# Attention with V as the stationary operand and P divided on GpSimd; expert stage with projections, values and three pieces of wo @ w1 between its units

## The chip, the cores and the metric

The kernel runs on one core of one Trainium2 chip. The time is device microseconds of that core for one execution, from the launch of the program to its end. PE is the matrix engine (TensorE), PEld its weight loads, DVE the vector engine, ACT the scalar engine, POOL is GpSimd, SP the engine whose queue issues all the DMAs here. PSUM is the memory that PE writes, SBUF the other on-chip memory; GpSimd reads SBUF alone.

## The reference

Three layers follow one another: a sparse attention with 8 heads, a mixture of 4 experts (each one causal head of attention, two experts for each position), and a block that mixes positions at rank 32 and then runs a wide two-layer network.

```python
# B, H, S, D = 2, 8, 768, 64
scores = q @ k.T / sqrt(D) + bias            # keys kept: the first n_global = 8 and the last n_local = 96
a = softmax(scores); x = a @ v               # x: 2 x 768 x 512
# experts: E = 4, K = 2 kept, head of 64
logits = x @ w_gate; w = softmax over the two largest
for e in range(E):
    a = causal_softmax((x @ wq[e]) @ (x @ wk[e]).T / 8)
    out += w[e] * (a @ (x @ wv[e]) @ wo[e])
# last block
u = out + (U V along the positions)
result = u + relu(u @ w_ch1) @ w_ch2
```

## The kernel before, in words

All of it is written out by hand: each engine has one program, in the order in which it is written, and semaphores are the only links. An engine that waits holds everything behind it.

**First attention.** 8 pairs of heads (p) times 6 tiles of 128 queries (i) are 48 units u. Two units are a duo d, so 24 duos, three to a pair. A unit has two halves s (the two heads, `par`). A half takes 128 queries against at most 256 keys: the tile's own 128 and a block of 128 made of the first 32 keys and the last 96 of the tile before. The steps are: `scores` on PE (line 1002 for tiles 0 and 1, lines 1004 and 1005 for 32 and 224 keys of the others), `attend` on DVE (L655: adds the bias, scales, keeps the minimum, writes `prob`), the exponential on ACT (`exp_step`, L460), `inverse` on DVE (1 / sum), `transposes` of P on PE (L1019, into `ps_t`), `evac` of the transposed P on ACT (L469), `values` on PE (L1038: P stationary, 64 columns of V moving, into `ps_o`), `scale_out` on DVE (L679, times 1 / sum), `x_turn` on PE (L1046, transposes back), `x_out` on DVE (L690 and L692, x as a rounded part `xh` and a rest `xl`). The loops of the engines run over d and hold their lag in their indices:

```python
# PE                                   # DVE                        # ACT
scores(2d), scores(2d+1)               x_out(d-4)                   evac(2d-2), evac(2d-1)
transposes(2d-2), transposes(2d-1)     scale_out(d-3)               four exp of duo d
values(d-2)                            four attend of duo d
x_turn(d-3)                            inverse(d-1)
```

SP loads each pair's q and k (two buffers, so pair p waits until all the scores of pair p-2 are done) and its V. Behind pair 2 come the weights; `load_weights(2)` and `load_weights(3)` wait until GpSimd has made the low parts `wqk_l` of what lay in their buffer before (`wl_done`).

**Expert stage.** wo is transposed on PE (L1174). `project(pp)` makes k and q of one pair of experts for one batch (pp = 0 to 3) with matmuls of split operands (L985, three products each); `project_hi` on ACT and `project_lo` on DVE write k as `mkh` + `mkl` and q as `mqs`, and SP copies halves of them to the other partitions. `project_values` makes all 12 tiles of values before the first unit. 24 units v = 6 pp + i follow, unit i with i + 1 tiles of keys: `m_scores` (L1130), `m_attend` (DVE, L655), `m_exp` (ACT, L460), `m_normalise` (DVE, L700 to L711), `m_transposes` (PE, L1146), `mevac` (ACT, L517), `m_values` (PE, L1162). PE runs scores two units ahead. `project(1)` to `project(3)` come whole, after units 0, 6 and 12.

**Last block.** `natural` (L1210) turns the experts' output, `both_weights(j)` makes wo @ w1 in 8 pieces between the small steps of the mixing, and from 298 us on `hidden` and `second` run over 2 x 16 tiles of the wide network.

## Time and profile before

| | |
|---|---|
| three runs | 520.68, 529.01 and 536.24 us, median 529.01 |
| profiled execution | 521.91 us, of which the span of the trace is 520.1 |
| PE busy | 483.1 us (93%) |
| DVE, ACT, POOL busy | 228.5, 187.6, 80.2 us (44%, 36%, 15%) |
| granted TensorE clock | 0.98 of full speed |
| DMA | 34.54 MB, 66 GB/s |

The page gives for each engine the time in which at least one instruction ran. 1.8 us of the profiled time lie around the span. The stages of the span: first attention to 117 us, experts to 265 us, preparation of the last block to 298 us, the wide network to the end.

### The profile page before, as it was taken

How to read it: one execution, taken by the hardware profiler on the slowest of the kernel's cores; microseconds unless marked ns; L12 is line 12 of the kernel's file. 1: busy time of each engine (PE TensorE's matmuls, PEld its weight loads, DVE VectorE, ACT ScalarE, POOL GpSimd, SP SyncE). 2: the span in 40 equal slices, each digit the busy share in tenths (PEclk: the TensorE clock that was granted, in tenths of full speed). 3: DMA queues.
4: the chain of work that ended last, by engine and by line, in shares of the span. 5: the costliest groups of instructions: out<-in, count | busy, mean ns of one | idle time of the engine just before them, and what ended most of it. 6: DMA issues, size and time to landing. Idle time of an engine off the chain costs nothing.

```text
span 520.1 us, 8734 instructions
## 1 busy us (share of the span) xinstructions
PE 483.1 (93%) x3368; PEld 420.2 (81%) x3368; DVE 228.5 (44%) x710; ACT 187.6 (36%) x485; POOL 80.2 (15%) x57
## 2 busy tenths in 40 slices
PE   2999999989996888978799999999999999999997
PEld 1888888869984776857589988888888788888886
DVE  3477766643479658375815512222222212222212
ACT  1676777733044557456833311111111211111112
POOL 0023300000005200050025201111122101111110
PEclk9999999988998999979999999999999999999999
DMA  6946333002015020130021101111111113211103
GB/s 224 288 120 202 113 113 113 1 1 62 1 27 164 33 61 2 32 112 1 2 82 42 39 23 41 42 42 40 42 42 41 42 38 84 81 62 42 40 1 121
DMA packets 20842, 34.54 MB, mean 66 GB/s; under 512 B 5216, under 2 KB 8160, under 8 KB 20800
## 3 DMA queue, kind: packets, MB, share of 16 engines
q1 hardware_dynamic: 20800, 33.97, 21.9%
q8 instruction: 27, 0.44, 0.3%
q14 instruction: 15, 0.12, 0.1%
HBM read 27.67 MB, written 3.15 MB: 59 GB/s over the span
## 4 chain that ended last, share of the span: by engine, by line
PE 84%; DVE 8%; ACT 3%; issue 3%; DMA 1%; SPq 0%; DVEq 0%; ACTq 0%
PE ps_s L985 25%; PE ps_o L985 16%; PE ps_t L985 13%; PE ps_o L1038 7%; PE ps_t L1019 5%; PE ps_o L1162 3%; PE ps_s L1005 3%; PE ps_t L1146 3%; DVE prob L655 3%; PE ps_s L1130 2%; PE ps_s L1004 2%; ACT prob L460 1%; PE ps_s L1002 1%; PE ps_o L1046 1%; ACT probT L517 1%
## 5 line engine op out<-in xcount | busy, mean ns | idle before, releaser
L610 ACT ACTIVATE hidh<-ps_o 128x768 fp32r<-128x768 f32 x32 | 26.0, 812 | 181.4 <-PE ps_o L985 181.4
L460 ACT ACTIVATE prob<-prob,smin 128x256 f32<-128x256 f32 (+3 forms) x144 | 77.2, 543 | 28.0 <-DVE smin L655 28.0
L968 DVE SCALAR_TENSOR_TENSOR hidl<-ps_o,hidh 128x768 fp32r<-128x768 f32 x32 | 30.6, 958 | 95.0 <-ACT hidh L610 95.0
L419 POOL TENSOR_TENSOR fl<-fraw,fh 128x512 fp32r<-128x512 f32 x32 | 41.3, 1291 | 177.6 <-DVE fh L897 177.6
L985 PE MATMUL ps_s<-hidh,fl 128*128 128x512 f32 x128 | 50.5, 394 | 0.0
L985 PE MATMUL ps_s<-hidl,fh 128*128 128x512 f32 x128 | 50.2, 392 | 0.0
L985 PE MATMUL ps_s<-hidh,fh 128*128 128x512 f32 x128 | 50.1, 391 | 0.0
L897 DVE CAST fh<-fraw 128x512 fp32r<-128x512 f32 x32 | 13.6, 426 | 71.5 <-PE ps_t L985 71.5
L985 PE MATMUL ps_o<-xl,w01h 128*128 128x256 f32 (+1 forms) x128 | 43.3, 338 | 0.0
L985 PE MATMUL ps_o<-xh,w01h 128*128 128x256 f32 (+1 forms) x128 | 43.2, 338 | 0.0
L985 PE MATMUL ps_o<-xh,w01l 128*128 128x256 f32 (+1 forms) x128 | 43.1, 337 | 0.0
L1146 PE MATMUL ps_t<-ident,prob 128*128 128x128 f32 x168 | 26.6, 293 | 16.3 <-DVE prob L711 8.2
L1146 PEld LDWEIGHTS ps_t<-ident,prob 128*128 128x128 f32 x168 | 19.6, 149 | 21.6 <-DVE prob L711 10.0
L1038 PE MATMUL ps_o<-vN,probT 128*128 128x64 f32 x224 | 37.0, 276 | 0.0
L985 PE MATMUL ps_t<-hidh,fh 128*128 128x256 f32 x128 | 36.1, 282 | 0.0
L985 PE MATMUL ps_t<-hidl,fh 128*128 128x256 f32 x128 | 36.0, 281 | 0.0
L985 PE MATMUL ps_t<-hidh,fl 128*128 128x256 f32 x128 | 35.7, 279 | 0.0
L469 ACT ACTIVATE probT<-ps_t 128x512 f32<-128x512 f32 (+1 forms) x48 | 25.4, 560 | 27.3 <-PE ps_t L1019 26.9
L655 DVE CUSTOM_DVE_ANT_0 prob<-ps_s,bias 128x256 f32<-128x256 f32 (+1 forms) x96 | 32.9, 397 | 3.5 <-PE ps_s L1005 3.1
L517 ACT ACTIVATE probT<-ps_t 128x512 f32<-128x512 f32 (+3 forms) x64 | 25.6, 448 | 23.8 <-PE ps_t L1146 23.6
L655 DVE CUSTOM_DVE_ANT_0 prob<-ps_s,causal 128x128 f32<-128x128 f32 (+5 forms) x48 | 28.0, 620 | 9.3 <-PE ps_s L1130 9.1
L1038 PEld LDWEIGHTS ps_o<-vN,probT 128*128 128x128 f32 x224 | 31.4, 196 | 0.0
(175 smaller groups left out, 1096.1 us busy)
## 6 DMA issues: line engine op xcount, KB each, us to landing
fraw<-in_w SPq DMA_DIRECT2D x32, 256.0 KB, 2.6
wraw<-in_w SPq DMA_DIRECT2D x8, 512.0 KB, 3.7
qT<-in_q SPq DMA_DIRECT2D x8, 384.0 KB, 3.2
kT<-in_k SPq DMA_DIRECT2D x8, 384.0 KB, 3.8
vN<-in_v SPq DMA_DIRECT2D x8, 384.0 KB, 4.8
out<-prob SPq DMA_DIRECT2D x12, 256.0 KB, 2.6
vB<-in_v SPq DMA_DIRECT2D x8, 192.0 KB, 5.0
mkh<-mkh SPq DMA_DIRECT2D x8, 192.0 KB, 2.6
```

The lines of the kernel that those rows point to most:

```text
L419: return pool.tensor_tensor(lo, raw, hi.bitcast(F32), ALU.subtract)
L460: act.activation(prob_s, prob_s, ACT.Exp, bias=smin[:, col:col + 1], scale=-1.0, accum_out=ssum[:, col:col + 1]).then_inc(done, 1)
L469: act.activation(a_probT[u % 4][:, :, 0:w], ps_t[:, u % 2, 0:2 * w].rearrange("p (a n) -> p a n", a=2), ACT.Copy).then_inc(evac_done, 1)
L517: act.activation(probT[:, v % 2, par, j0 * P:j1 * P], ps_t[:, g % 2, 0:(j1 - j0) * P], ACT.Copy).then_inc(mevac_done, 1)
L610: act.activation(hidh[:, f % 2, :], ps_o[:, 0:S], ACT.Relu).then_inc(hidh_done, 1)
L655: dve.tensor_tensor_reduce(out=dst, in0=src, in1=mask, scale=-SCALE, scalar=3e38, op0=ALU.add, op1=ALU.min, accum_out=smin[:, col:col + 1] ...
L968: dve.scalar_tensor_tensor(hidl[:, f % 2, :], ps_o[:, 0:S], 0.0, hidh[:, f % 2, :].bitcast(F32), ALU.max, ALU.subtract).then_inc(hidl_done, 1)
L985: last = pe.matmul(dst, a, m, start=start and k == 0, stop=stop and k == n - 1, **kw)
L1005: last = pe.matmul(ps_s[:, s % 4, FIRST:2 * P], q, k[:, (i - 1) * P + FIRST:(i + 1) * P], start=True, stop=True)
L1019: last = pe.transpose(ps_t[:, u % 2, (n * par + j) * P:(n * par + j + 1) * P], a_prob[s % 8][:, j * P:(j + 1) * P], ident[:, :])
L1038: last = pe.matmul(ps_o[:, at:at + 64], a_probT[u % 4][:, par, n * P:(n + 1) * P], v, start=n == 0, stop=n == (i > 0), skip_group_check=True)
L1146: last = pe.transpose(ps_t[:, g % 2, (j - j0) * P:(j - j0 + 1) * P], m_prob[r % 6][:, j * P:(j + 1) * P], ident[:, :])
```

## The change

In the first attention V is now the stationary operand and the transposed P moves, so that x comes out with its channels on partitions and needs no turn (`x_turn`, `scale_out` and `xn` are gone). 1 / sum therefore has to be in P before it is transposed: GpSimd adds the epsilon (`safe`) and multiplies the four halves of a duo (`divide`). The 256 keys of a tile now lie side by side in `kT` (five DMAs instead of one, and a copy of the first 32 keys on GpSimd, `first`), so a half's scores are one matmul. Three of four `evac` go to DVE, ACT writes `xh` (`x_hi`), DVE `xl` (`x_lo`). GpSimd's low parts of the weights come in eight halves behind the divisions of duos 4 to 11.

In the expert stage q and k stay in plain float32 (`mq`, `mk`; no low parts, no copies by DMA), the projections for pp = 1 to 3, the values of the second batch and the pieces 0 to 2 of wo @ w1 are cut into 18 pieces that PE runs between the units by the table `FILL`, all into one bank (`ps_fill`), and DVE takes them out between its own steps. The first five tiles of w1 are split by ACT and DVE instead of GpSimd.

```diff
+FILL = [(-1, 1, "p", (1, "k")), (0, 0, "p", (1, "q")), (0, 1, "p", (1, "rest")), (1, 0, "v", NT), (1, 1, "v", NT + 1),
...
+        (12, 1, "p", (3, "q")), (13, 1, "p", (3, "rest")), (18, 1, "w", 0), (19, 1, "w", 1), (20, 1, "w", 2)]
+GATES_1_AT = 10
+W1_AT = {4: 0, 8: 1, 10: 2, 14: 3, 16: 4}
...
+def by_act(u):
+    return u % 4 == 0
...
# SP
-                sp.dma_start(kT[:, p % 2, :], t["k"][b, pr]).then_inc(qk_in[p], 16)
+                sp.dma_start(kT[:, p % 2, 0:2 * P], t["k"][b, pr, :, 0:2 * P]).then_inc(qk_in[p], 16)
+                for i in range(2, NT):
+                    sp.dma_start(kT[:, p % 2, 2 * P * (i - 1) + FIRST:2 * P * i],
+                                 t["k"][b, pr, :, P * (i - 1) + FIRST:P * (i + 1)]).then_inc(qk_in[p], 16)
...
                 load_pair(2)
                 load_weights(1)
+                load_pair(3)
                 load_weights(2)
-                load_pair(3)
                 load_weights(3)
...
# GpSimd
+            def first(p):
+                slot = kT[:, p % 2, :].rearrange("p (i n) -> p i n", i=NT - 1)
+                pool.wait_ge(qk_in[p], QK_IN)
+                pool.tensor_copy(slot[:, 1:NT - 1, 0:FIRST],
+                                 slot[:, 0:1, 0:FIRST].broadcast_to([P, NT - 2, FIRST])).then_inc(first_keys, 1)
+            def safe(d):
+                pool.wait_ge(exp_done, 4 * d + 4)
+                pool.tensor_scalar(seps[:, four], ssum[:, four], EPS, None, ALU.add).then_inc(safe_done, 1)
+            def divide(d):
+                pool.wait_ge(inv_done, d + 1)
+                for s in range(4 * d, 4 * d + 4):
+                    pool.tensor_scalar(x, x, sinv[:, s:s + 1], one[:, 0:1], ALU.mult, ALU.mult).then_inc(norm_done, 1)
...
+                for d in range(N_DUO + 1):
+                    if d % X_PARTS == 0 and d // X_PARTS + 1 < B * HP:
+                        first(d // X_PARTS + 1)
+                    if 1 <= d <= N_DUO:
+                        safe(d - 1)
+                        divide(d - 1)
+                    if 5 <= d < 5 + 8:
+                        weight_lo(d - 5)
...
# ACT
+                for d in range(N_DUO + 4):
+                    if 3 <= d < N_DUO + 3 and by_act(2 * (d - 3)):
+                        evac(2 * (d - 3))
                     if d < N_DUO:
                         for s in range(4 * d, 4 * d + 4):
...
+                    if d >= 4:
+                        x_hi(d - 4)
...
+            take_queries()
+            m_exp(0)
+            m_exp(1)
+            gates_exp(0)
+            for v in range(M_UNIT + 2):
...
+                if v < M_UNIT:
+                    mevac(v)
+                fill_hi(v, 0)
+                if v + 2 < M_UNIT:
+                    m_exp(v + 2)
...
+                if v in W1_AT:
+                    w1_hi(W1_AT[v])
...
# DVE
                 for d in range(N_DUO + 4):
-                    if d >= 4:
-                        x_out(d - 4)
                     if 3 <= d < N_DUO + 3:
-                        scale_out(d - 3)
+                        for u in (2 * (d - 3), 2 * (d - 3) + 1):
+                            if not by_act(u):
+                                evac(u)
                     if d < N_DUO:
...
-                        for s in range(4 * d, 4 * d + 4):
-                            attend(s)
+                        attend(4 * d)
+                        attend(4 * d + 1)
                     if 1 <= d <= N_DUO:
                         inverse(d - 1)
+                    if d < N_DUO:
+                        attend(4 * d + 2)
+                        attend(4 * d + 3)
+                    if d >= 4:
+                        x_lo(d - 4)
...
+            for v in range(M_UNIT + 1):
+                if v + 1 < M_UNIT:
+                    m_normalise(v + 1)
+                fill_take(v - 1, 1)
+                fill_take(v, 0)
+                if v + 2 < M_UNIT:
+                    m_attend(v + 2)
+                if v == GATES_1_AT:
+                    gates(1)
+                if v in W1_AT:
+                    w1_lo(W1_AT[v])
...
# PE
+                    pe.matmul(a_score[s % 8][:, 0:keys.stop - keys.start], qT[half, p % 2, i * P:(i + 1) * P],
+                              kT[half, p % 2, keys], start=True, stop=True, skip_group_check=True).then_inc(s_done, 1)
...
+                            last = pe.matmul(ps_o[half, at:at + P], v, a_probT[u % 4][:, par, n * P:(n + 1) * P],
+                                             start=n == 0, stop=own, skip_group_check=True)
...
-                    if 1 <= d <= N_DUO:
-                        transposes(2 * d - 2)
-                        transposes(2 * d - 1)
+                    if d >= 3:
+                        values(d - 3)
                     if 2 <= d < N_DUO + 2:
-                        values(d - 2)
-                    if d >= 3:
-                        x_turn(d - 3)
+                        transposes(2 * d - 4)
+                        transposes(2 * d - 3)
...
             for v in range(M_UNIT + 1):
+                if v < M_UNIT:
+                    m_transposes(v)
+                fill(v, 0)
                 if v + 2 < M_UNIT:
                     m_scores(v + 2)
-                if v and v % NT == 0:
+                if v:
                     m_values(v - 1)
...
+                fill(v, 1)
```

**The order on DVE** in the middle of the first attention, one duo, before. `xh`, `xl` and `xn` are x_out and scale_out of older duos, the four `prob,smin` rows with 256 columns are `attend`, L671 and L673 are `inverse`.

```order
L690 CAST xh<-ps_o 128x256 [waits a_xt]
L692 TENSOR_TENSOR xl<-ps_o,xh 128x256 [waits a_xh]
L679 TENSOR_TENSOR xn<-ps_o,sinv 128x256 [waits a_inv,a_pv]
L655 ISA prob,smin<-ps_s,bias 128x256 [waits a_t,a_s]
...
L655 ISA prob,smin<-ps_s,bias 128x256 [waits a_t,a_s]
...
L671 TENSOR_SCALAR seps<-ssum 128x4 [waits a_exp]
L673 RECIPROCAL sinv<-seps 128x4 [waits a_inv]
```

The same duo after; L751 is `evac`, L733 `attend`, L758 `inverse`, L765 `x_lo`.

```order
L751 COPY probT<-ps_t 128x512 [waits a_pv,a_t]
L733 ISA prob,smin<-ps_s,bias 128x256 [waits a_t,a_s]
...
L733 ISA prob,smin<-ps_s,bias 128x256 [waits a_t,a_s]
...
L758 RECIPROCAL sinv<-seps 128x4 [waits a_safe]
L733 ISA prob,smin<-ps_s,bias 128x256 [waits a_t,a_s]
...
L733 ISA prob,smin<-ps_s,bias 128x256 [waits a_t,a_s]
...
L765 TENSOR_TENSOR xl<-ps_o,xh 128x256 [waits a_xh]
```

The write of `xl` moved from ahead of the duo's attends, where it waited for PE, to behind them, where it waits for ACT (`a_xh`). **The order on ACT**, before and then after, of two duos (four exponentials, `prob`, to a duo):

```order
L469 ACTIVATE probT<-ps_t 128x2x128 [waits a_pv,a_t]
L469 ACTIVATE probT<-ps_t 128x512 [waits a_pv,a_t]
L460 ACTIVATE prob,ssum<-prob,smin 128x256 [waits a_sub] x4
L469 ACTIVATE probT<-ps_t 128x512 [waits a_pv,a_t] x2
L460 ACTIVATE prob,ssum<-prob,smin 128x256 [waits a_sub] x4
```

```order
L532 ACTIVATE probT<-ps_t 128x512 [waits a_pv,a_t]
L523 ACTIVATE prob,ssum<-prob,smin 128x256 [waits a_sub] x4
L539 ACTIVATE xh<-ps_o 128x256 [waits a_pv]
L523 ACTIVATE prob,ssum<-prob,smin 128x256 [waits a_sub] x4
L539 ACTIVATE xh<-ps_o 128x256 [waits a_pv]
```

A write of `xh` now stands behind each duo's four exponentials, which themselves wait for the duo's attends (`a_sub`). **The order on GpSimd** after, around duo 8 (before there was nothing here but a split of a whole weight about every 8 us): the second half of a weight's low part (`wqk_l`), the first keys of pair 4, and then a duo's `safe` and `divide`.

```order
L441 TENSOR_TENSOR wqk_l<-wraw,wqk_h 128x2x256 [waits wh_done]
L463 COPY kT<-kT 128x4x32 [waits qk_in4]
L470 TENSOR_SCALAR seps<-ssum 128x4 [waits a_exp]
L478 TENSOR_SCALAR prob<-prob,sinv,one 128x256 [waits a_inv]
L478 TENSOR_SCALAR prob<-prob,sinv,one 128x256 x3
```

What moved in is the whole of it; the copy of pair 4's first keys stands ahead of duo 8's `safe`. **The order on SP** after, at the same place:

```order
L356 DMA wraw<-in_wv 128x4x256 [waits wl_done]
L357 DMA wraw<-in_w_gate 128x4x4
L353 DMA wraw<-in_wo 128x1024 [waits wl_done]
L323 DMA qT<-in_q 128x768 [waits a_s]
L324 DMA kT<-in_k 128x256
L326 DMA kT<-in_k 128x224 x4
```

The loads of pair 4 (the last three rows) stand behind the load of wo, which waits for the second `wl_done`.

## Rows read from the trace of the kernel before

**Rows 1.** Windows: stretch, its length, busy time of each engine, clock, DMA.
```profile
58.88:71.03 12.15, 12.15 (x114) 10.76 (x114) 8.62 (x40) 8.80 (x32) 1.81 (x1) 1.00 0.37 126
...
117.00:265.45 148.45, 128.67 (x977) 108.10 (x976) 92.82 (x286) 74.99 (x188) 17.05 (x10) 0.94 0.16 44
```

**Rows 2.** Chain of waits, attention and its end: start, duration, what.
```profile
46.73 0.86 PE ps_s L1002 x8
47.59 1.02 PE ps_t L1019 x8
48.61 1.73 PE ps_o L1038 x16
...
117.04 1.71 PE ps_t L1174 x8
```

**Rows 3.** Chain of waits, expert stage: values, the gates' first and last step, m_values.
```profile
127.82 2.88 PE ps_t L985 x24
...
146.79 0.17 DVE ggt L836
...
149.41 0.20 DVE gate L853
...
179.22 1.24 PE ps_o L1162 x20
```

**Rows 4.** Timeline, ACT: two exponentials in a row.
```profile
66.05 0.50 ACT L460 ACTIVATE prob<-prob,smin 128x256 f32<-128x256 f32 x1
...
66.54 0.50 ACT L460 ACTIVATE prob<-prob,smin 128x256 f32<-128x256 f32 x1
```

**Rows 5.** Timeline, DVE: attends of 256 and of 512 columns in a row.
```profile
64.22 0.42 DVE L655 CUSTOM_DVE_ANT_0 prob<-ps_s,bias 128x256 f32<-128x256 f32 x1
...
64.57 0.42 DVE L655 CUSTOM_DVE_ANT_0 prob<-ps_s,bias 128x256 f32<-128x256 f32 x1
...
158.81 0.69 DVE L655 CUSTOM_DVE_ANT_0 prob<-ps_s,causal 128x512 f32<-128x512 f32 x1
...
159.43 0.69 DVE L655 CUSTOM_DVE_ANT_0 prob<-ps_s,causal 128x512 f32<-128x512 f32 x1
```

**Rows 6.** Timeline: the first attend and the first exponential, 128 columns.
```profile
11.48 0.29 DVE L655 CUSTOM_DVE_ANT_0 prob<-ps_s,bias 128x128 f32<-128x128 f32 x1
...
11.81 0.40 ACT L460 ACTIVATE prob<-prob,smin 128x128 f32<-128x128 f32 x1 [2.44 <-DVE smin L655]
```

**Rows 7.** Groups by form: ACT's copy of 256 columns, GpSimd's operations; count, busy, mean ns.
```profile
L469 ACT ACTIVATE probT<-ps_t 128x256 f32<-128x256 f32 x8 | 3.1, 384 | 11.9 <-PE ps_t L1019 11.9
...
L419 POOL TENSOR_TENSOR fl<-fraw,fh 128x512 fp32r<-128x512 f32 x32 | 41.3, 1291 | 177.6 <-DVE fh L897 177.6
...
L419 POOL TENSOR_TENSOR wqk_l<-wraw,wqk_h 128x1024 fp32r<-128x1024 f32 x4 | 9.4, 2360 | 35.5 <-DVE wqk_h L722 35.3
L445 POOL CAST xh<-wraw 128x1024 fp32r<-128x1024 f32 x6 | 6.4, 1060 | 141.4 <-DMA wraw<-in_w 97.8 <-PE ps_s L985 43.6
```

**Rows 8.** SP's issues and the time to landing of a pair's keys.
```profile
16.43 0.42 SPq L316 DMA_DIRECT2D wraw<-in_wq  x1
...
44.61 0.43 SPq L292 DMA_DIRECT2D kT<-in_k  x1
...
kT<-in_k SPq DMA_DIRECT2D x8, 384.0 KB, 3.8
```

**Rows 9.** Timeline: a DVE operation beside one of GpSimd, both on SBUF.
```profile
161.46 3.69 DVE L711 TENSOR_SCALAR prob<-prob,wgt 128x384 f32<-128x384 f32 x2
...
161.49 2.34 POOL L419 TENSOR_TENSOR xl<-wraw,xh 128x1024 fp32r<-128x1024 f32 x1
```

**Rows 10.** Groups by form, expert stage: attend, exponential and division of 768 columns.
```profile
L655 DVE CUSTOM_DVE_ANT_0 prob<-ps_s,causal 128x768 f32<-128x768 f32 x8 | 7.4, 954 | 1.2 <-PE ps_s L1130 1.1
L460 ACT ACTIVATE prob<-prob,smin 128x768 f32<-128x768 f32 x8 | 7.4, 933 | 0.0
...
L711 DVE TENSOR_SCALAR prob<-prob,wgt 128x768 f32<-128x768 f32 x8 | 4.6, 617 | 0.1
```

More of the change, by code:

```diff
@@ L433, in _ @@
+            with pool.Else():
+                for n in range(8):
+                    weight_lo(n)
             pool.wait_ge(wh_done, 5)
@@ L880, in m_normalise, with w01_lo @@
                           gate[:, NT * b + i, 2 * pr:2 * pr + 2])
-            for v in range(M_UNIT + 2):
-                if v < M_UNIT:
-                    m_attend(v)
-                if v in GATES_AT:
-                    gates(GATES_AT[v])
-                if 1 <= v <= M_UNIT:
-                    m_normalise(v - 1)
-                if v - 2 in PROJECT_AT:
-                    project_lo(PROJECT_AT[v - 2])
+            def w01_lo(j):
+                src = ps_fill if j < W1_IN_FILL else ps_s[:, j % 4, :]
+                dve.wait_ge(w01h_done, j + 1)
+                dve.tensor_tensor(w01l[j], src.rearrange("p (c n) -> p c n", c=EP), w01h[j].bitcast(F32),
+                                  ALU.subtract).then_inc(w01l_done, 1)
@@ new lines, in _, with w1_lo @@
+            m_attend(0)
+            m_attend(1)
+            gates(0)
+            m_normalise(0)
+            def w1_lo(j):
+                dve.wait_ge(w1h_done, j + 1)
+                dve.tensor_tensor(by_unit(w1l[j]), w1_raw(j), by_unit(w1h[j]).bitcast(F32),
+                                  ALU.subtract).then_inc(w1l_done, 1)
+            for v in range(M_UNIT + 1):
[5 more added lines that the diff above has]
+                    m_attend(v + 2)
+                if v == GATES_1_AT:
+                    gates(1)
+                if v in W1_AT:
+                    w1_lo(W1_AT[v])
@@ new lines, in project_values, with both_weights @@
+            def project_values(n):
+                if n >= 4:
+                    pe.wait_ge(v_out, 2 * (n - 3))
+                values_of(n, ps_v[n % 4][:, 0:260]).then_inc(v_done, 1)
+            def both_weights(j, dst):
+                pe.wait_ge(w1l_done, j + 1)
+                for pr in range(EP):
+                    w = slice(pr * P, (pr + 1) * P)
+                    last = split_product(dst[:, pr * W1N:(pr + 1) * W1N],
+                                         [(woT_h[:, c, w], woT_l[:, c, w], w1h[j % W1S][:, c, :], w1l[j % W1S][:, c, :])
+                                          for c in range(KT)], skip_group_check=True)
+                return last
@@ new lines, in fill_emptied, with fill @@
+            def fill_emptied(n):
+                _, _, kind, x = FILL[n]
+                if kind == "w":
+                    pe.wait_ge(w01l_done, x + 1)
+                elif kind == "v":
+                    pe.wait_ge(v_out, 2 * (x + 1))
+                elif x[1] == "q":
+                    pe.wait_ge(q_out, 2 * x[0])
+                elif x[1] == "k":
+                    pe.wait_ge(k_out, 2 * x[0])
+                else:
+                    pe.wait_ge(q_out, 2 * x[0] + 1)
+            def fill(v, place):
+                for n in fills(v, place):
+                    _, _, kind, x = FILL[n]
+                    if n == 0:
+                        pe.wait_ge(v_out, 2 * 4)
+                    else:
+                        fill_emptied(n - 1)
+                    if kind == "v":
+                        last = values_of(x, ps_fill[:, 0:260])
+                    elif kind == "w":
+                        last = both_weights(x, ps_fill)
+                    elif x[1] == "rest":
+                        projected(ps_fill[:, 0:256], x[0] // EP, x[0] % EP, 0, HI)
+                        last = projected(ps_fill[:, 256:512], x[0] // EP, x[0] % EP, 1, HI)
+                    else:
+                        last = projected(ps_fill, x[0] // EP, x[0] % EP, x[1] == "q", LO)
+                    last.then_inc(fill_done, 1)
@@ L1161, in m_values @@
                         e = slice(HD * (2 * pr + par), HD * (2 * pr + par + 1))
[L1162 removed]
+                        last = pe.matmul(ps_o[half, i % 3 * P:(i % 3 + 1) * P], mv[:, b, j, e],
                                          probT[:, v % 2, par, j * P:(j + 1) * P], start=j == 0, stop=j == i,
```

480 lines of the change are left out of this document (221 added, 259 removed).

## The prediction, made before the result was known

> **What bounds the kernel now.** The windows come first. In the first attention PE is busy without a gap: one pair of heads takes 12.15 us and PE is busy for all of them, DVE for 8.6, ACT for 8.8, GpSimd for 1.8 [rows 1]. The chain of waits shows of what a pair is made: per duo 0.86 us of scores for tiles 0 and 1, about 1.0 of transposes and 1.73 of values [rows 2]. In the expert stage PE is busy for 128.7 of 148.5 us at a mean clock of 0.94, so some 20 us are waits and a few more are slow matmuls [rows 1]. The wide network behind is PE alone and isn't touched. So there are two questions: what bounds attention once PE needs less, and how much of the 20 us goes.
>
> **Attention, what PE saves.** A matmul of values goes as two instructions. Before, one with 128 stationary and 64 moving columns took 1.73 / 16 = 0.108 us; the experts' values, which already have 64 stationary and 128 moving columns, take 1.24 / 20 = 0.062 [rows 2, 3]. A pair has 44 of them: 4.75 us become 2.7. The scores of tiles 2 to 5 lose their extra matmul of 32 keys and should take what tiles 0 and 1 take, 0.86 a duo. With 2.9 of transposes and no x_turn a pair needs PE for 3 x 0.86 + 2.9 + 2.7 = 8.2 us, 4 less than now. On one page's rule this would be less: the Trainium skill (TensorEngine Tiling, Tiling Modes) says that a change of tiling mode drains TensorE, and the changed kernel goes between whole array and column halves twice in every duo. The experts' rows hold such a change in their 1.24 us, so it is at most 0.2, and nothing below rests on it.
>
> **Attention, what takes PE's place.** DVE and ACT are handed to each other once in every duo, in an order that admits no overlap: four attends, four exponentials, then `x_hi` on ACT, then `x_lo` on DVE, then DVE's `evac`, then the next duo's attends. Exponentials follow one another at 0.49 us [rows 4]. Attends at 0.35 for 256 columns and 0.62 for 512 [rows 5]; I take the latter for an `evac` of 512 columns, which also reads PSUM once, and 0.35 for `x_lo`. From the start of an attend to its exponential it is 0.33 us at 128 columns, so 0.47 at 256 [rows 6]. `x_hi` is ACT's copy of 256 columns, 0.38 [rows 7]. A duo is then 0.47 + 4 x 0.49 + 0.38 + 0.35 = 3.16 us and one `evac` (3.8) or two (4.4), in turn; the 128-column halves of tiles 0 and 1 take 0.4 to 0.6 off one duo in three. Over a period of six duos I get 23.7 us, **11.8 a pair, against 12.15 now**. PE's 8.2 lie below it, and so does DVE's own work, some 8.1 (12 attends 3.9, evacs 2.6, the rest 1.6). PE's own loop through DVE (evac, values, transposes: 1.2 + 0.1 + 1.9 = 3.2 a duo) is shorter too.
>
> **GpSimd.** No row shows its tensor_scalar with two operands by partition. From below, the cast: 1.06 us at 1024 columns; from above, the tensor_tensor: 2.36 at 1024 and 1.29 at 512, so 0.2 fixed [rows 7]. At 256 columns that is 0.41 to 0.75 us; I take 0.5, nearer the cast, since it too has one large operand. Four and `safe` are 2.2 us a duo (3.2 at most), with half a weight's low part 3.5 (4.5). Under 3.9 it hides; at the upper end it costs 0.6 in each of 8 duos, 5 us. The Trainium skill (GPSIMD Engine Reference, section 3.1) gives 1.03 to about 1.8 cycles an element for one-input loops; its estimate for 256 columns would be 0.2 to 0.4 us and the fixed part, which agrees with the rows.
>
> **Attention, waits that come in.**
> (a) Start. SP now issues four more loads ahead of `rel` and `kpos`, 0.47 us each [rows 8], and the attends wait for `kpos`: they begin at 13.4 instead of 11.5 [rows 6].
> (b) GpSimd's `first(2)` stands ahead of `safe(2)` and waits for pair 2's keys. Before, SP was through with its constants at 16.9 [rows 8]; with 8 more issues it is at 20.5, and the six loads of q and k go out until 23.2. The last lands some 2.6 later, at 26. DVE reaches `inverse(2)` at about 20.8 and holds there to 26.6: 5.8 us. Duo 4 begins on DVE at 27.7 and duo 6 at 36.9 (4.4 + 3.8 and 1.0 for a bias and a cast).
> (c) From duo 6 to the end of duo 23: 3 x 23.7 = 71.0, plus casts and biases that no longer hide under PE, 3.0. These read and write SBUF alone, and such an operation waits for GpSimd's: one took 3.7 us beside a tensor_tensor of 2.3 [rows 9]. With operations of 0.5 on GpSimd I add 0.25 for each of six, 1.5.
> (d) Pair 4's keys are queued on SP behind wo's load, which waits for the second `wl_done`, and that now comes when GpSimd is through with duo 7 and a weight's second half, 5.5 us into DVE's duo 8. Then 3.2 of issue and 3 to landing, behind 0.5 MB of wo: 12. DVE wants `safe(8)` at 6.3. That is 6 us, once. For pairs 3 and 5 to 7 the keys land 5.2 us after the scores that they wait for (2.7 of issue, 2.6 of landing; a pair's keys in one load took 3.8 [rows 8]) and `inverse` comes at 5.5 to 6, so they cost nothing.
> (e) Tail: last evacs, values and transposes in turn, 7.5 us from the end of duo 23.
> Sum: 36.9 + 71.0 + 3.0 + 1.5 + 6.2 + 7.5 = 126 for the transposes of wo, which begin at 117.0 now [rows 2]: **9 us later**. If (b) and (d) both fail to come it is 114, 3 earlier.
>
> **Experts.** Ahead of the first unit six tiles of values go, 1.44 us each [rows 3], and q and k are one copy each instead of hi, lo and a DMA: the part shrinks by 8.6, from 31.4 to 22.8 us (transposes of wo 1.7, first projection 9.1, values 8.6, two scores 0.9, the first piece 2.5). In the loop PE now has its old work, those 8.6 us and three pieces of wo @ w1 at 2.85, another 8.55. As a floor, all of PE's waits go: 106 us of PE in the loop, in which I leave 2 us a pair of experts for the transposes that wait for ACT's evacuation, and 5 at its head, since `gates(0)` (2.8 us on DVE [rows 3]) and `m_normalise(0)` stand between the last values and the first transposes and the first piece's copy waits behind them. That makes 111. From above, DVE and ACT hand over here too: `m_normalise(v + 1)` and `m_attend(v + 2)` alternate on DVE with the exponential between them exposed. For 768 columns that is 0.6 for three small steps (0.2 each, as the gates' 13 in 2.8) and 2 x 0.55 of division, 0.87 of one attend, 0.12, and 2 x 0.88 of exponential and 0.15, 4.6 us, against some 3 of PE's at tile 3 [rows 10]; each of five splits of w1 adds 2.2 to it, and `mevac(v)` stands behind the exponentials of v + 1, so the transposes of tiles 4 and 5 wait. Following the loop unit by unit with such numbers gives 127.5. I take the middle, 119. The stage: 22.8 + 119 = 142 against 148.4, **6.6 less** (15 less to 2 more).
>
> **Preparation of the last block.** Three pieces fewer, 8.55; they covered the small steps, of which I leave 2 us bare: **6.5 less** (4.5 to 8.5).
>
> **Sum.** +9 - 6.6 - 6.5 = -4 us. The profiled execution took 521.9, so **518 us**. That is 11 below the median of the three runs shown, which spread by 3%, so the percentages below are against 521.9. About 2% either way is what a measurement can tell from no change.
>
> **Rivals.**
> *The handover doesn't bind.* If ACT gets to `x_hi` early or DVE's steps overlap more than I read, attention falls to PE's and DVE's 8.2 a pair: 3.6 less for 6.7 pairs, 24 us, and with the experts at their floor 8 more: **486**. For it: no engine is full. Against it: the order is fixed and every link has a row. 0.15.
> *The experts' loop runs near its floor,* attention as forecast: 518 - 8 = **510**. For it: the pieces fill just the units with few keys, in which PE waited. Against it: DVE's cycle of 4.6. 0.12.
> *GpSimd becomes the bound, slower.* It decides from 0.93 us for a half (4 x 0.93 + 0.2 = 3.94) and from 0.61 in duos 4 to 11. If the two-scalar form costs what a tensor_tensor of 512 does, 1.29, a duo takes 5.4: 1.4 x 20 and 1.3 x 8 more, 38 us, **556**; at 0.9 it would be 9 us, 527. For it: no row bounds a two-scalar form. Against it: both rows that there are stay under 0.76. 0.12 for the whole of it.
> *The clock.* PE is busy for 8.2 of 11.8 us with a pause in every duo. Over the experts now, with pauses, the clock was 0.94 [rows 1], so some of it went at the lower of the two levels. At that level PE needs 5.4 us a duo, more than 3.9, and is the bound: 1.5 x 20, **548**. Against it: in attention now, with the same transposes in between, the clock is full [rows 1]. 0.06.
> *No gain in the experts and all the new waits,* 127.5 in the loop and 5 for GpSimd at its upper bound: 518 + 8.5 + 5 = **531**. 0.1.
>
> **Numbers.** The forecast's own case (508 to 526) has 0.45. The range leaves out the two slow rivals at 548 and more and a little of the fast one: 487 to 536. Faster by over 2% (under 511.5): the first rival, most of the second and a slice of my own case, 0.35. Slower by over 2% (above 532): 0.22. Within: 0.43.
>
> **What would show it.** In the profile after: a pair takes 11.8 us and PE waits in it for DVE's `probT`; DVE's `xl` waits for ACT's `xh` by 1.2 us a duo; GpSimd's half takes 0.5; two holes of PE of some 6 us at 20 and at duo 8; the transposes of wo near 126; the loop of the units 119 long. I am wrong if a pair takes 9 us or less, if GpSimd is busy for most of attention, or if PE's clock is at its lower level there.

## The result, and the profile after

The changed kernel takes **547.2 us** (median of four runs, 544.3 to 550.0), the one before 525.8 on the same chip (520.7 to 536.2): a ratio of 1.047, 95% interval 1.039 to 1.054. It is slower, and 518 was forecast in a range up to 536. The profiled execution took 550.0 (span 548.1), against 521.9 (520.1).

The windows of the changed kernel, with the columns of [rows 1]: attention, three stretches of 10 us in it, the expert stage, and of that the loop over the units.

```profile
12.00:140.20 128.20, 82.74 (x704) 62.29 (x704) 72.55 (x287) 60.39 (x227) 71.02 (x136) 0.85 0.38 112
...
40.00:50.00 10.00, 5.01 (x36) 3.93 (x34) 6.97 (x21) 4.19 (x15) 7.97 (x14) 0.66 0.30 89
...
60.00:70.00 10.00, 2.80 (x25) 2.25 (x24) 3.95 (x17) 2.80 (x11) 5.11 (x11) 0.67 0.32 100
...
100.00:110.00 10.00, 7.56 (x74) 5.47 (x71) 5.13 (x23) 5.67 (x23) 5.30 (x12) 1.00 0.54 166
...
140.20:300.20 160.00, 137.53 (x1051) 107.94 (x1049) 85.79 (x290) 69.98 (x182) 7.55 (x5) 0.94 0.08 27
...
161.95:300.16 138.21, 115.74 (x902) 88.32 (x901) 78.17 (x262) 65.87 (x171) 7.51 (x5) 0.93 0.07 24
```

Three stages make the difference of 28.0 us between the spans. The transposes of `wo` begin at 140.3 instead of 117.0 [rows 2]: **attention is 23.2 us longer**. From there to the first transposes of the last block it is 159.9 instead of 148.4 [rows 1]: **the experts are 11.5 longer**. From there to the end it is 247.9 instead of 254.7: **the preparation is 6.7 shorter**. Before, PE was busy for nearly all of attention (102 of the 105 us from 12 to 117); now it is busy for 83 of 128 us, and its clock there is 0.85.

What attention waits for, by the view of waits from 12 to 140 us (engine, tile and line, what it waited for: us in all, times, the longest):

```profile
PE ps_o L1135 <- DVE probT L751: 41.6, 19, 7.2
...
POOL kT L463 <- DMA kT<-in_k: 28.6, 7, 8.6
...
DVE xl L765 <- ACT xh L539: 24.8, 20, 1.3
DVE sinv L758 <- POOL seps L470: 23.7, 9, 7.7
```

The second and the fourth row are one thing. GpSimd copies a pair's first keys (`first`) and waits there for the DMA; `safe` stands behind it, and DVE's `inverse` waits for `safe`. The timeline of DVE and of GpSimd shows the two longest places, and, between them, one of those that had been put at nothing:

```profile
26.08 0.18 DVE L758 RECIPROCAL sinv<-seps 128x4 f32<-128x4 f32 x1 [5.21 <-POOL seps L470]
...
40.63 0.18 DVE L758 RECIPROCAL sinv<-seps 128x4 f32<-128x4 f32 x1 [2.60 <-POOL seps L470]
...
63.95 0.29 POOL L463 COPY kT<-kT 128x128 f32<-128x128 f32 x1 [8.63 <-DMA kT<-in_k]
...
64.59 0.18 DVE L758 RECIPROCAL sinv<-seps 128x4 f32<-128x4 f32 x1 [7.70 <-POOL seps L470]
```

The chain of waits of the changed kernel: PE's transposes and scores at its lower level, and its transposes at full clock; one duo at full clock that hands over from DVE to ACT and back; the head of the experts' loop, where the division and the copy of the keys end what PE waits for; and a split of `w1`, ACT's part and DVE's.

```profile
70.26 1.90 PE ps_t L1115 x8
72.16 1.84 PE ps_s L1102 x8
...
79.16 1.02 PE ps_t L1115 x8
...
112.09 2.08 ACT prob L523 x8
114.17 0.28 ACT xh L539
...
114.47 0.04 DVE xl L765
...
114.81 0.26 DVE probT L751
...
116.01 0.41 DVE prob L733
...
165.43 0.62 DVE prob L784 x2
166.05 0.61 DVE mk L975
...
219.39 0.95 ACT xh L617
...
220.37 1.23 DVE xl L987
```

GpSimd's operations by form: a half of 256 columns takes 0.562 us, and four of them with `safe` some 2.5 of a duo's 4 us.

```profile
L478 POOL TENSOR_SCALAR prob<-prob,sinv,one 128x256 f32<-128x256 f32 x80 | 43.8, 562 | 18.3 <-DVE sinv L758 18.3
```

### The profile page after: what moved, and what is told of

Read it like the earlier page. It is cut to its first block, busy times and chain, and to the rows that moved or that the text cites. A ratio compares the mean times of both kernels' runs of the same rounds, so it can differ in the third digit from the quotient of the medians.

```text
span 548.1 us, 8485 instructions
## 1 busy us (share of the span) xinstructions
PE 465.7 (85%) x3192; PEld 385.3 (70%) x3192; DVE 224.0 (41%) x676; ACT 170.5 (31%) x463; POOL 123.8 (23%) x180
## 4 chain that ended last, share of the span: by engine, by line
PE 68%; DVE 9%; ACT 8%; issue 6%; DMA 4%; SPq 3%; POOL 1%; DVEq 0%; ACTq 0%; POOLq 0%
PE ps_s L1085 22%; PE ps_o L1085 18%; PE ps_t L1085 10%; ACT prob L523 6%; DMA kT<-in_k 4%; PE ps_s L1256 3%; PE ps_o L1287 3%; PE ps_o L1135 3%; PE ps_t L1115 3%; PE ps_t L1272 3%; DVE probT L751 2%; SPq L326 2%; PE ps_s L1102 1%; DVE prob L733 1%; PE ps_o L1359 1%
## 5 line engine op out<-in xcount | busy, mean ns | idle before, releaser
L478 POOL TENSOR_SCALAR prob<-prob,sinv,one 128x256 f32<-128x256 f32 (+1 forms) x96 | 50.9, 546 | 25.7 <-DVE sinv L758 25.7
L1007 DVE CAST fh<-fraw 128x512 fp32r<-128x512 f32 x32 | 14.2, 444 | 71.8 <-PE ps_t L1085 71.2
L1272 PE MATMUL ps_t<-ident,prob 128*128 128x128 f32 x168 | 26.3, 292 | 19.3 <-ACT probT L580 14.1
L1085 PE MATMUL ps_o<-xh,w_late 128*128 128x512 f32 (+1 forms) x160 | 42.4, 337 | 0.0
L1135 PE MATMUL ps_o<-probT,vB 128*64 128x128 f32 x128 | 15.3, 312 | 30.6 <-DVE probT L751 29.7
L508 POOL CAST xh<-wraw 128x1024 fp32r<-128x1024 f32 x3 | 3.1, 1042 | 156.2 <-DVE prob L784 156.2
L1102 PE MATMUL ps_s<-kT,qT 64*128 64x256 f32 (+1 forms) x192 | 29.1, 426 | 9.6 <-DMA kT<-in_k 8.2
L733 DVE CUSTOM_DVE_ANT_0 prob<-ps_s,bias 128x256 f32<-128x256 f32 (+1 forms) x96 | 34.0, 392 | 1.7 <-PE ps_s L1102 1.0
L1135 PEld LDWEIGHTS ps_o<-probT,vB 128*64 128x64 f32 x128 | 8.9, 151 | 36.3 <-DVE probT L751 21.0
L1135 PE MATMUL ps_o<-probT,vN 128*64 128x128 f32 x224 | 24.0, 318 | 11.9 <-DVE probT L751 11.9
L1115 PE MATMUL ps_t<-ident,prob 128*128 128x128 f32 x176 | 30.9, 326 | 2.0 <-POOL prob L478 1.9
## 6 DMA issues: line engine op xcount, KB each, us to landing
wraw<-in_w SPq DMA_DIRECT2D x8, 512.0 KB, 3.3
```

Source lines behind the costliest of these rows:

```text
L478: pool.tensor_scalar(x, x, sinv[:, s:s + 1], one[:, 0:1], ALU.mult, ALU.mult).then_inc(norm_done, 1)
L733: dve.tensor_tensor_reduce(out=dst, in0=src, in1=mask, scale=-SCALE, scalar=3e38, op0=ALU.add, op1=ALU.min, accum_out=smin[:, col:col + 1] ...
L1085: last = pe.matmul(dst, a, m, start=start and k == 0, stop=stop and k == n - 1, **kw)
L1102: pe.matmul(a_score[s % 8][:, 0:keys.stop - keys.start], qT[half, p % 2, i * P:(i + 1) * P], kT[half, p % 2, keys], start=True, stop=True, ...
L1115: last = pe.transpose(ps_t[:, u % 2, (n * par + j) * P:(n * par + j + 1) * P], a_prob[s % 12][:, j * P:(j + 1) * P], ident[:, :])
L1135: last = pe.matmul(ps_o[half, at:at + P], v, a_probT[u % 4][:, par, n * P:(n + 1) * P], start=n == 0, stop=own, skip_group_check=True)
```

## Experiments on attention

Every ratio is to the kernel before on the same chip. "Attention ends" is the start of the transposes of `wo` in the profiled execution.

**The copies of the first keys later** (`keys_late`). They move behind the division of a pair's third duo:

```
-                    if d % X_PARTS == 0 and d // X_PARTS + 1 < B * HP:
-                        first(d // X_PARTS + 1)
                     if 1 <= d <= N_DUO:
                         safe(d - 1)
                         divide(d - 1)
+                    if d % X_PARTS == 2 and d // X_PARTS + 1 < B * HP:
+                        first(d // X_PARTS + 1)
```

> Only GpSimd's copies of the first keys move: each now stands behind the division of the third duo of a pair instead of ahead of the first, five to eight microseconds later, when the keys have landed. If the waits for the keys are what cost attention its 23 us (they hold DVE's inverse for 23.7 us in nine waits), the transposes of wo come at about 120 instead of 140.3 and the kernel takes 525 to 530. If TensorE's low clock is what costs, and PE at 5.7 us a duo is the bound between the waits, the end moves by 5 to 8 us only (540) and the clock in attention stays near 0.85. If only the handover between DVE and ACT bound, nothing but the two longest waits (13 us) would go: 534.

Measured: 528.9 us, ratio 1.010 (1.006 to 1.013); attention ends at 119.1. The waits of `inverse` fall from 23.7 to 2.8 us, and attention by 21.1; DVE still waits 25.3 us for `xh`. The place of one call was worth 18 us in the median; of the ratio of 1.047 it left 1.010. The windows of attention, and then DVE's wait for `safe` in it:

```profile
12.00:119.10 107.10, 79.95 (x704) 59.72 (x705) 70.93 (x286) 59.78 (x227) 71.23 (x136) 0.89 0.46 133
```

```profile
DVE sinv L758 <- POOL seps L470: 2.8, 6, 1.0
```

**The handover opened** (`x_early`). ACT takes `x_hi(d - 4)` ahead of the duo's exponentials, DVE `x_lo(d - 4)` between the halves of its attends:

```
+                    if d >= 4:
+                        x_hi(d - 4)
                     if d < N_DUO:
                         for s in range(4 * d, 4 * d + 4):
...
-                    if d >= 4:
-                        x_hi(d - 4)
...
                     if 1 <= d <= N_DUO:
                         inverse(d - 1)
+                    if d >= 4:
+                        x_lo(d - 4)
                     if d < N_DUO:
                         attend(4 * d + 2)
                         attend(4 * d + 3)
-                    if d >= 4:
-                        x_lo(d - 4)
```

> Only the handover between DVE and ACT is opened: ACT takes x_hi ahead of the duo's exponentials and DVE takes x_lo between the halves of the duo's attends. The handover theory says that a duo falls from 3.9 to some 3.0 us wherever the clock is full, and the waits for the keys stay: attention ends 10 to 15 us earlier, 532 to 537. The clock theory says that the duos at 5.7 us (PE at its lower level) stay as long, and only those at full clock gain: 3 to 6 us, 541 to 544. DVE's xl should wait for ACT's xh hardly at all (26 us before the edit).

Measured: 538.4 us, ratio 1.024 (1.016 to 1.032), attention ends at 130.6, 9.6 earlier. The time lies between the two ranges of the expectation. DVE no longer waits for `xh` (24.8 us before the edit), but for `safe` it now waits 36.9 us instead of 23.7: it comes there sooner and finds the keys no earlier. So over half of what the handover gave back went into the other wait.

```profile
DVE sinv L758 <- POOL seps L470: 36.9, 16, 8.5
```

**Both** (`keys_x`).

> Both edits together. If waits and handover are the cause and the low clock only follows from them (PE pauses, and the clock falls), PE is busy nearly without a pause, the clock of attention returns to 0.95 or more and a duo takes 3.0 us: the transposes of wo at 95 to 105 and the kernel at 505 to 512. If the clock falls for another reason (the many short matmuls of 64 rows or columns), PE still needs 5.7 us a duo in half of attention: wo near 118, 525.

Measured: **510.9 us, ratio 0.973** (0.965 to 0.981), attention ends at 102.3. Alone the edits gave 21.1 and 9.6 us, together 37.9. The clock is 0.98, with the same short matmuls of 64 rows and columns as before. The first fence is the window of attention, the second the chain of waits from 65 us on. Behind the handover GpSimd comes next: four divisions, the copy of the keys and `safe` follow one another on the chain, so the gain over `keys_late` is 16.8 and not the 24 of the rival "the handover doesn't bind".

```profile
12.00:102.30 90.30, 74.55 (x705) 55.44 (x705) 68.97 (x288) 61.42 (x227) 72.40 (x136) 0.98 0.54 158
```

```profile
65.24 2.17 POOL prob L478 x4
67.42 0.24 POOL kT L463
...
67.74 0.23 POOL seps L470
...
70.47 1.09 PE ps_o L1135 x16
71.56 1.02 PE ps_t L1115 x8
72.58 1.11 PE ps_s L1102 x8
```

**PE kept busy, four runs.** Spare matmuls of the identity go into the bank that the scores then overwrite; `values` and all else stay.

```
                         pe.wait_ge(sub_done, s - 8 + 3)
+                        for _ in range(6 if s >= 16 else 0):
+                            pe.matmul(a_score[s % 8][:, 0:P], ident[:, :], ident[:, :], start=True, stop=True,
+                                      skip_group_check=True)
```

The line runs for both heads of a unit, so the first run had twelve a duo (its expectation says six), and the later ones, with 2 and 1 in place of the 6, four and two.

> The changed kernel with six matmuls of the identity (128 columns, about 0.21 us each at full clock) ahead of each duo's scores from duo 4 on, into the bank that the scores then overwrite; they change nothing in the result and fill the pause of 1.9 us that PE has in each duo. The clock theory with the pauses as its cause: the granted clock of attention rises from 0.85 to 0.95 or more, and attention ends no later than 140 and up to 10 us earlier although PE has 25 us more to do: 537 to 547. If the pauses have nothing to do with the clock, it stays at 0.85, PE needs 5.7 plus up to 2.5 us in each slow duo and attention ends 20 us later: 565.

Twelve: 575.4 us, ratio 1.094 (1.085 to 1.103); attention ends at 165.5 and its clock is 0.98. Each spare matmul took 0.24 us, so PE itself was the bound, at 5.8 to 6.6 us a duo, and the time lies outside both forecasts of the expectation.

> The changed kernel with four spare matmuls a duo instead of twelve (the run before had twelve, 0.24 us each: its clock was full, but PE at 6.0 us a duo had itself become the bound). Four are 0.96 us: PE needs 2.86 + 0.96 = 3.8 us at full clock, just under the pitch of 4.1 to 4.3 that the changed kernel has where its clock is full. The waits for the keys stay. If the pauses are what lowers the clock: clock of attention 0.93 or more, the duos between the waits at 4.1 to 4.4 instead of 5.7, the transposes of wo 5 to 12 us earlier than 140.2, the kernel at 535 to 542. If the clock has another cause: 0.85 as before, PE at 5.7 + 1.9 in the slow duos, attention ends 10 to 20 us later, 557 to 567.

Four: 557.3 us, 1.063 (1.051 to 1.075); attention ends at 150.8. In the long waits for keys PE stood still here too, and the clock fell behind them (0.62 from 50 to 60 us); from 110 to 140 us, with only short ones, it was 1.00. The mean of attention is 0.89. The run doesn't decide.

> The kernel with the copies of the first keys moved (528.9, no wait for keys, handover kept, a pause of PE in each duo, clock of attention 0.89, wo at 119.1) with the four spare matmuls a duo. Without the long waits only the pauses of the handover are left to lower the clock, so this is the clean test: if they do, the clock rises to 0.97 or more and PE, busy for 3.8 of 4.1 us, costs nothing: attention ends at 112 to 119, the kernel at 522 to 530. If the clock has another cause it stays at 0.89 and attention ends 10 or more later, 538 to 550.

Four, on top of `keys_late`: 533.8 us, 1.016 (1.010 to 1.022); attention ends at 126.1. The clock is 1.00 in every stretch from 30 to 110 us, where `keys_late` had 0.84 to 0.96 from 20 to 70 us. So with the pauses filled the clock doesn't fall. Pauses as such don't lower it, though: from 70 to 110 us `keys_late` has one in every duo too, none longer than 1.4 us up to 106 us, and its clock there is 1.00; its longer ones, up to 2.9 us, lie before 60 us, and so does most of the low clock. In the run with four PE had no pause left from 60 to 110 us and was the bound again; the time lies between the two forecasts of the expectation.

> The kernel with the copies of the first keys moved (528.9, attention ends at 119.1 at a mean clock of 0.89) with two spare matmuls a duo, 0.48 us. With four the clock was full from 30 to 110 us, but PE then had no pause left and was itself the bound (126.1). Two leave it below the handover's 4.0 us a duo at full clock. If the low clock costs time in this kernel: the clock rises to 0.95 or more and attention ends at 113 to 117, the kernel at 523 to 527. If the low clock only stretches matmuls inside the pauses and costs nothing: 118 to 120 whatever the clock is, 528 to 530.

Two: 532.3 us, 1.014 (1.006 to 1.022); attention ends at 120.9 in the profiled run, against 119.1 without them. (The profiled run, 528.4, is the quickest of the five; the others took 531.3 to 532.6.) The windows are all of attention and the stretch from 20 to 71 us; behind them stand the same stretch of `keys_late`, and then the `inverse` of duo 13, first in this run and then in `keys_late`:

```profile
12.00:120.90 108.90, 99.11 (x784) 73.24 (x784) 71.55 (x286) 59.89 (x227) 70.79 (x136) 0.97 0.45 131
...
20.00:71.00 51.00, 46.09 (x376) 33.95 (x374) 36.41 (x134) 27.09 (x102) 37.75 (x67) 1.00 0.57 171
```

```profile
20.00:71.00 51.00, 37.91 (x332) 28.46 (x330) 36.46 (x134) 26.96 (x103) 38.02 (x67) 0.88 0.58 174
```

```profile
71.04 0.17 DVE L758 RECIPROCAL sinv<-seps 128x4 f32<-128x4 f32 x1
```

```profile
71.07 0.17 DVE L758 RECIPROCAL sinv<-seps 128x4 f32<-128x4 f32 x1
```

The clock is full where it was 0.88, DVE and ACT do the same work in the same time, and DVE reaches the `inverse` of duo 13 at the same moment: up to there the lower clock of `keys_late` only stretched matmuls inside PE's pauses. The 1.8 us by which attention is longer come later, between 75 and 110 us, where `keys_late` had the full clock too and PE with the spare matmuls has no pause left.

There is one place in attention where the lower level does cost time, its end. Behind the last duo DVE waits for PE, and the clock is below full from there on in `keys_late` (0.64) and in this run (0.69) alike. In the changed kernel a duo's transposes lie there on the chain and take 1.83 us instead of 1.02:

```profile
133.41 1.83 PE ps_t L1115 x8
```

A mean clock of 0.89 over 107.1 us means 23.6 us at the lower level; the Trainium skill (TensorE: Matmul & The Clock Gate, HAM oscillation) prices such time at half; the estimate from it is 11.8 us. Raising the mean to 0.97 won none of it.

## Experiments on the expert stage

They stand on top of `keys_x`; its stage takes 158.9 us, that of the changed kernel 159.9.

**The keys' piece taken ahead of the gates** (`keys_before_gates`).

```
-FILL = [(-1, 1, "p", (1, "k")), (0, 0, "p", (1, "q")), (0, 1, "p", (1, "rest")), (1, 0, "v", NT), (1, 1, "v", NT + 1),
+FILL = [(-1, 1, "p", (1, "k")), (-1, 1, "p", (1, "q")), (0, 1, "p", (1, "rest")), (1, 0, "v", NT), (1, 1, "v", NT + 1),
...
             m_attend(1)
+            dve.wait_ge(fill_done, 1)
+            dve.tensor_copy(mk[:, 1, LO], ps_fill).then_inc(k_out, 1)
             gates(0)
```

> On top of the two edits of attention (510.9): DVE copies the first filled piece (keys of experts 2 and 3) ahead of the gates instead of behind gates and division, and PE makes the queries of these experts there too, ahead of the first transposes. The theory that the head of the loop has a hole of 7.2 us on PE (chain: gates 2.8, division 2.2, copy 0.6) and a slow matmul of 5.3 us behind it says: the hole shrinks by 2.9 and the slow piece returns to 2.9: the expert stage 153 to 155 instead of 158.9, the kernel at 505 to 507. The rival: DVE's and ACT's cycle of some 4.6 us a unit sets the stage and gives nothing back, 510.

Measured: 506.6 us, 0.968 (0.961 to 0.974), the stage 155.0. In the changed kernel PE waited 2.75 us for the division and 1.39 for the copy, and then ran the next piece at its lower level; here the piece waits 0.78 us for the copy and then runs at full speed. First rows of PE's timeline in the changed kernel, then in this one:

```profile
159.19 0.39 PE L1085 MATMUL ps_o<-xh,wqk_h 128*128 128x512 f32 x1
...
164.87 0.43 PE L1272 MATMUL ps_t<-ident,prob 128*128 128x128 f32 x2 [2.75 <-DVE prob L784]
166.70 0.80 PE L1085 MATMUL ps_o<-xh,wqk_h 128*128 128x512 f32 x1 [1.39 <-DVE mk L975]
167.29 0.63 PE L1085 MATMUL ps_o<-xl,wqk_h 128*128 128x512 f32 x1
```

```profile
123.96 0.51 PE L1089 MATMUL ps_o<-xh,wqk_h 128*128 128x512 f32 x1 [0.78 <-DVE mk L984]
124.30 0.40 PE L1089 MATMUL ps_o<-xl,wqk_h 128*128 128x512 f32 x1
```

**The splits of w1 on GpSimd** (`w1_gpsimd`): `W1_AT` is empty, and GpSimd takes all eight pieces, without its wait for the last division.

> On top of the two edits of attention (510.9): the first five splits of w1 go to GpSimd, which is idle in the expert stage, instead of ACT and DVE (0.95 + 1.23 us each, on the chain at three of five places). The theory that the splits lie on the chain between exponentials and division: three holes shrink by 2.2 each and the clock behind them rises, the stage 150 to 154, the kernel at 502 to 506. The rival: DVE's operations wait for GpSimd's (one took 3.7 us beside a tensor_tensor of 2.3 in the kernel before), five times up to 3.4 us on DVE's side of the same chain: no gain or up to 5 us slower, 511 to 516.

Measured: 512.3 us, 0.979 (0.972 to 0.986), the stage 159.3: no gain. DVE is rid of five splits of 1.23 us and yet busy for 86.7 us instead of 85.7: its 48 divisions alone take 22.6 us instead of 19.6. Their group, and then from the timeline the two divisions of unit 3 beside a tensor_tensor of GpSimd, which take 0.88 us in `keys_x`, and a DVE operation of two columns beside another, which takes 0.16 us otherwise:

```profile
L785 DVE TENSOR_SCALAR prob<-prob,wgt 128x128 f32<-128x128 f32 (+5 forms) x48 | 22.6, 512 | 0.9
```

```profile
147.07 3.05 DVE L785 TENSOR_SCALAR prob<-prob,wgt 128x512 f32<-128x512 f32 x2
147.10 2.34 POOL L441 TENSOR_TENSOR xl<-wraw,xh 128x1024 fp32r<-128x1024 f32 x1
...
215.80 2.35 POOL L441 TENSOR_TENSOR wqk_l<-wraw,wqk_h 128x1024 fp32r<-128x1024 f32 x1
...
215.99 2.17 DVE L780 TENSOR_TENSOR wgt<-sinv,gate 128x2 f32<-128x2 f32 x1
```

Behind those two divisions DVE takes a piece of the values out of `ps_fill` (`logit`), and PE waits 3.5 us for it, a wait that `keys_x` doesn't have.

**The three pieces of wo @ w1 back in the preparation** (`no_pieces`): the three `"w"` entries leave `FILL`, and the order of the preparation is that of the kernel before.

> On top of the two edits of attention (510.9): the three pieces of wo @ w1 leave the expert loop again and go back into the preparation, in the order that the kernel before has there. If they filled pauses of PE, the stage keeps its 158.9 and the preparation grows by 6: 517. If they only moved (PE had no pause at units 18 to 20), the stage shrinks by 8.6 and the preparation grows by 6 to 8.6: 509 to 511.

Measured: 512.0 us, 0.977 (0.971 to 0.984). The stage is 4.8 shorter (154.1), what follows it 6.3 longer. So of 8.6 us of pieces 3.8 had filled pauses. In the median the pieces are worth 1.2 us, which is less than the spread of `keys_x` (510.0 to 513.6); the time lies between the two forecasts of the expectation. PE is busy for 129.1 us in this stage, as it was before the change (128.7 [rows 1]), yet the stage takes 5.7 more: the new loop loses that even without the pieces.

```profile
102.20:256.30 154.10, 129.13 (x979) 99.39 (x977) 83.45 (x287) 68.10 (x179) 0.00 (x0) 0.93 0.08 25
```

**The splits in the shortest units** (`w1_small`, on top of `keys_before_gates`).

```
-W1_AT = {4: 0, 8: 1, 10: 2, 14: 3, 16: 4}
+W1_AT = {4: 0, 5: 1, 10: 2, 16: 3, 17: 4}
```

> On top of keys and queries ahead of the gates (506.6, stage 155.0): the splits of w1 move from units 4, 8, 10, 14, 16 to 4, 5, 10, 16, 17, in which the next attends and exponentials are those of tiles 0 and 1, the shortest. If the splits lie on the chain at units 8 and 14 (0.95 + 1.23 us each, between an exponential and a division): two times 2.2 less and a little for the clock, stage 149 to 151, kernel 501 to 503. If the chain has something else waiting there (ACT's probT behind the exponentials), 505 to 507.

Measured: **502.4 us, 0.958** (0.954 to 0.962), the stage 150.0, its clock 0.97. It is the fastest of all, ahead of both kernels.

```profile
102.20:252.20 150.00, 133.81 (x1051) 105.15 (x1049) 85.29 (x290) 69.84 (x182) 6.06 (x4) 0.97 0.09 29
```

**Evacuations ahead of exponentials** (`evac_first`, on top of `keys_before_gates`). The waits of PE in the stage pointed here: for ACT's `probT` 14.1 us in the changed kernel, 6.3 before the change.

```
                     mevac(v)
+                if v % NT >= 4 and v + 1 < M_UNIT:
+                    m_exp(v + 1)
                 fill_hi(v, 0)
-                if v + 2 < M_UNIT:
+                if v + 2 < M_UNIT and (v + 1) % NT < 4:
                     m_exp(v + 2)
```

> On top of keys and queries ahead of the gates (506.6): in the units of tiles 4 and 5 ACT moves the transposes out before it takes the next unit's exponentials. PE's second group of transposes waits for that 13.6 us in eight places (6.3 us in nine in the kernel before). If this order is what the loop lost against the kernel before: those waits fall to some 5 us and the stage to 146 to 150, kernel 498 to 502. The rival: the exponentials now come later by 1 to 2 us, so DVE's division and the next transposes wait by what was won: 504 to 509.

Measured: 513.6 us, 0.979 (0.975 to 0.984), 7 us slower than its base. PE waits only 7.0 us for `probT`, and 13.5 (before the edit 3.2) for DVE's division, whose exponentials now come late. Both forecasts of the expectation were too fast. The wait was a place at which the chain shows, not a cost by itself.

```profile
PE ps_t L1278 <- DVE prob L786: 13.5, 8, 2.8
PE ps_t L1278 <- ACT probT L580: 7.0, 8, 3.1
```

**Both edits of the loop** (`evac_w1`).

> Both edits of the expert loop together on top of keys and queries ahead of the gates. If both lie on the same chain at different units, they add: stage 143 to 147, kernel 494 to 499. If either only shifts the wait to the other, no better than the better of the two.

Measured: 512.0 us, 0.977 (0.972 to 0.981). They don't add; the order of ACT costs more than the splits give.

## Why the prediction was wrong, step by step

*The handover* held, and PE stayed below it. A duo's values take 1.09 us at full clock and its scores 1.11 (the chain of `keys_x`). The sum had 0.86 for the scores, read from the duo of tiles 0 and 1, but tile 0 has only 128 keys. By these numbers PE needs an estimated 9.0 us a pair and not 8.2, which changes nothing under a bound of 12. A pair's pitch at full clock, without a wait for keys, was 12.0 us (`inverse` at 112.32 and 128.26, four duos of 3.99), against 11.8. DVE waited 24.8 us in 20 duos for ACT's `xh`, 1.24 each, against 1.2.

*GpSimd:* 0.562 us a half against 0.5, inside the bounds. The estimate from the Trainium skill (GPSIMD Engine Reference, section 3.1), 0.2 to 0.4 us, with the fixed part of 0.2 from the rows makes 0.4 to 0.6, and 0.562 lies in it. Its parts were off: 128 columns take 0.465, so the fixed part is 0.37 and 128 more columns cost 0.1. In the rival on GpSimd 4 x 0.93 + 0.2 is 3.92 and not 3.94; nothing hangs on it.

*(b)*, pair 2's keys, held: 5.8 forecast, 5.2 measured, `inverse(2)` at 26.1 against 26.6. *(d)* held for pair 4: 6.2 against 7.7.

**The step that failed** is the rest of (d): "For pairs 3 and 5 to 7 the keys land 5.2 us after the scores [...] so they cost nothing." They cost 2.6, 2.1, 1.8 and 1.9, or 8.6 with one more of 0.2. Both times that the step compared were off. Pair 7's loads began at 101.9 and the copy ran at 108.1, 6.2 us later and not 5.2; and `inverse` was there after 4.9 us, not after 5.5 to 6. Pair 4's wait was 1.5 longer than its 6.2. That makes 10.1 of the 14.2 us by which attention was missed, and `keys_late` shows that such waits are worth their whole length. The start doesn't count: `inverse` waited 1.2 and 1.0 there too, but (a) had the attends at 13.4 and they came at 12.1, and duo 6 began at 36.6 against 36.9. The tail (e) took 9.5 us and not 7.5, with PE at its lower level for part of it (8.0 in `keys_x`, at full clock). The last 2.4 lie in the duos, most of which took 5.0 to 5.9 us between 29 and 75 us. Up to 71 us the same duos are as long in `keys_late` as in `keys_late_busy2` with the clock full, so DVE's biases and casts make them long; but behind the longest wait of the changed kernel PE's 1.90 and 1.84 us stand on the chain, where full clock takes 1.02 and 1.11. That duo took 5.9 us against 5.3 in `keys_late`.

*The clock rival* had 548 us, and the run took 547, with the clock low as that rival said. **It was still not the cause, and its number fits by luck.** It put PE at its lower level on the chain in 20 duos, 30 us. The clock did fall with PE's pauses (`keys_late_busy4` shows the link). But with the waits gone it rose only from 0.85 to 0.89 and 21.1 of 23.2 us came back, and raising it to 0.97 brought nothing; what the lower level did cost in the changed kernel's attention is the small places named above. A rival whose number fits is not yet shown.

*The experts* were missed by 18 us (142 against 159.9). The part ahead of the loop was right, 21.7 against 22.8. **The loop was the second step that failed:** 138.2 us against 119, and against 127.5 at the upper bound. Two terms of it were too small. PE's own work was put at 106 and is 115.7. The old loop had 97.3 us of it, at a mean clock of 0.94:

```profile
148.40:265.45 117.05, 97.27 (x758) 78.39 (x757) 78.40 (x239) 68.47 (x173) 17.05 (x10) 0.94 0.17 48
```

With the 8.6 us of values and 8.55 of pieces that the prediction itself adds, that is 114.4. So 106 left out what the lower clock costs, or some of the work; how the 8 us divide isn't shown. Some 4 are the clock (the whole stage has 133.8 instead of 137.4 in `w1_small`, at 0.97). Its waits were put at 13 and are 22.5: the head (5 expected; `keys_before_gates` won 3.9 of it and of the slow piece behind it), the splits (5.0 won by moving three of them), and what PE waits for ACT's `probT`. That last part, 14.1 us in the changed kernel and still 12.5 in `w1_small`, was not resolved; `evac_first` shows only that this order of ACT isn't its remedy.

*The preparation:* 6.5 less forecast, 6.7 measured.

The errors, 14.2 + 17.9 - 0.2 = 31.9 us, make up the distance from the forecast's span (520.1 - 4 = 516) to 548.1.

## What to carry to other kernels

An engine that waits for a DMA with a small copy holds everything queued behind it: place such a copy where its data has long landed, not at the first point where it could run. Before a wait is called free, compare the two arrival times with the spread of both: here 5.2 against 5.5 to 6 us was a forecast of nothing, and the four places cost 8.4 us. And two edits that open waits on the same loop must be run together too: alone they gave 21 and 10 us, together 38.

## What the runs showed of the hardware

- TensorE's granted clock was 0.84 to 0.96 from 20 to 70 us in `keys_late`, with pauses of up to 2.9 us, and 1.00 there when two spare matmuls a duo took up most of them, with the same real work. From 70 to 110 us, with a pause in every duo but none over 1.4 us up to 106, it was 1.00 without spare matmuls.
- The lower level cost nothing where another engine was the bound (the `inverse` of duo 13 at 71.07 us at a clock of 0.88, at 71.04 at 1.00), and it did cost time where PE lay on the chain (a duo's transposes 1.83 us instead of 1.02 at the end of the changed kernel's attention).
- GpSimd's tensor_scalar with two operands by partition took 0.562 us for 256 columns and 0.465 for 128; by these two, 0.37 of it is fixed.
- DVE operations on SBUF stood still beside GpSimd's tensor_tensors: one of two columns took 2.17 us beside 2.35 of GpSimd, and the divisions 0.512 us in the mean of 48 instead of 0.451.
